# Attention, top-1 experts and a tanh layer in one kernel: all head pairs of a middle tile merged, softmax sums divided out later, weight splits moved

## The reference

```
# 1. attention: q, k, v of (4 batches, 8 heads, 768 rows, 64)
scores = q @ k.T / 8
keep   = (column < 4) | (0 <= row - column < 128)     # 4 sink keys, window of 128
a      = softmax(where(keep, scores, -1e9))           # + 1e-9 in the denominator
x      = (a @ v), heads side by side                  # 3072 x 512
# 2. one of 8 experts for each row
logits = x @ w_gate ; e = argmax(logits)
x      = softmax(logits)[e] * (relu(x @ w1[e]) @ w2[e])   # 512 -> 1024 -> 512
# 3. for all rows
h      = x @ w_in ; out = (h - tanh(h)) @ w_out       # 512 -> 2048 -> 512
```

## Time and profile before

| what | value |
|---|---|
| median of 3 runs | 1098.68 us (1098.45 to 1098.95) |
| the profiled execution's own time | 1091.45 us |
| its span in the profile | 1089.7 us |
| TensorE clock granted | 0.999 of full speed |
| busy in the span | PE 99%, PE weight loads 80%, DVE 56%, ACT 44%, POOL 44% |

### The profile page before, as it was taken

The page is one execution under the profiler, slowest core; times in us unless marked ns, Lnnn a source line. Parts: engine busy times, 40 slices in busy tenths (PEclk is TensorE's granted clock), DMA queues, the critical chain, the costliest instruction groups (busy, mean ns, idle before and its releaser), DMA issues.

```text
span 1089.7 us, 17185 instructions
## 1 busy us (share of the span) xinstructions
PE 1077.8 (99%) x6028; PEld 876.7 (80%) x6028; DVE 610.5 (56%) x1354; ACT 481.6 (44%) x1033; POOL 484.0 (44%) x492
## 2 busy tenths in 40 slices
PE   9999999999999999999999999999999999999997
PEld 6777876888888888888878888888888888888885
DVE  7778775233222332223378766666666666666664
ACT  7899875333142424442454433333333333333332
POOL 3265634715043617482264444345335335334532
PEclk9999999999999999999999999999999999999999
DMA  8646824516134434463231100101001011000000
GB/s 292 204 120 230 260 81 153 196 49 203 39 94 158 130 132 156 132 225 125 92 110 53 57 22 19 30 11 40 20 20 39 2 38 39 1 1 11 30 1 38
DMA packets 38204, 99.44 MB, mean 91 GB/s; under 512 B 8304, under 2 KB 8944, under 8 KB 33008
## 3 DMA queue, kind: packets, MB, share of 16 engines
q1 hardware_dynamic: 29392, 52.04, 15.4%
q0 software_dynamic: 8448, 46.17, 12.3%
q10 hardware_dynamic: 288, 0.26, 0.1%
HBM read 75.84 MB, written 22.61 MB: 90 GB/s over the span
## 4 chain that ended last, share of the span: by engine, by line
PE 97%; DVE 1%; issue 1%; ACT 1%; POOL 0%; POOLq 0%; ACTq 0%; DVEq 0%
PE bank L775 24%; PE bank L783 23%; PE bank L714 15%; PE bank L700 14%; PE bank L480 5%; PE bank L512 4%; PE bank L494 3%; PE bank L706 2%; PE bank L459 1%; PE bank L675 1%; PE bank L759 1%; PE bank L558 1%; PE bank L544 1%; PE bank L536 1%; DVE probT L1089 0%
## 5 line engine op out<-in xcount | busy, mean ns | idle before, releaser
L1521 POOL TENSOR_TENSOR weights<-raw,weights 128x1024 fp32r<-128x1024 f32 x70 | 166.6, 2400 | 199.3 <-ACT weights L843 198.2
L783 PE MATMUL bank<-weights,gT_hi 128*128 128x512 f32 x768 | 238.6, 392 | 0.3 <-DVE gT_lo L1388 0.3
L775 PE MATMUL bank<-mT_hi,weights 128*128 128x512 f32 x768 | 189.8, 389 | 0.7 <-ACT mT_hi L997 0.7
L1620 POOL TENSOR_SCALAR ser<-ser 128x512 f32<-128x512 f32 x96 | 61.8, 643 | 281.5 <-DVE ser L1333 281.4
L775 PEld LDWEIGHTS bank<-mT_hi,weights 128*128 128x128 f32 x768 | 144.1, 188 | 30.8 <-ACT mT_hi L997 0.9
L783 PEld LDWEIGHTS bank<-weights,gT_hi 128*128 128x128 f32 x768 | 142.6, 188 | 29.4 <-DVE gT_lo L1388 0.7
L783 PE MATMUL bank<-weights,gT_lo 128*128 128x512 f32 x384 | 149.6, 390 | 0.0
L1011 ACT ACTIVATE bank<-bank 128x512 f32<-128x512 f32 x96 | 55.9, 582 | 210.4 <-DVE ser L1364 210.4
L714 PE MATMUL bank<-weights,hT_hi 128*128 128x512 f32 x464 | 148.6, 401 | 0.0
L700 PE MATMUL bank<-weights,mT_hi 128*128 128x512 f32 x456 | 144.2, 397 | 0.0
L1622 POOL TENSOR_SCALAR sq<-sq 128x512 f32<-128x512 f32 x94 | 140.6, 1496 | 0.0
(11 more groups left out here) (164 smaller groups left out, 1593.7 us busy)
## 6 DMA issues: line engine op xcount, KB each, us to landing
raw<-w_all POOLq DMA_DIRECT2D x32, 1024.0 KB, 5.5
raw<-w_all SPq DMA_DIRECT2D x8, 1024.0 KB, 6.4
sorted_y<-ys SPq DMA_DIRECT2D x30, 257.0 KB, 4.2
xs<-sorted_x SPq DMA_DIRECT2D x29, 257.0 KB, 3.0
v_in<-vt SPq DMA_DIRECT2D x24, 256.0 KB, 3.9
kT<-kt SPq DMA_DIRECT2D x23, 264.0 KB, 3.1
qT<-qt SPq DMA_DIRECT2D x23, 256.0 KB, 4.1
raw<-sorted_y SPq DMA_DIRECT2D x20, 257.0 KB, 2.7
```

The source lines that it names most:

```text
L775: done = e.matmul(bank[HB[n % 3]][:, :], wt[:, f // 2, c, cols], x[:, c, :], start=(m == 0), stop=(m == 3 * CH - 1))
L783: done = e.matmul(bank[YB[i]][:, :], x[:, n % 3, rows], wt[:, f, :], start=(f == 0 and m == 0), stop=(f == GCH - 1 and m == 2))
L1521: e.tensor_tensor(lo, src, hi.bitcast(F32), ALU.subtract).then_inc(s_w_lo, 1)
L1620: e.tensor_scalar(row, row, SERIES_2, 1.0, ALU.mult, ALU.add).then_inc(s_ser, 1)
```

## The change

1. `is_merged` now holds for all four pairs of the middle tiles but those of tiles 22 and 23, which keep the old form; `part_on_act` is left for the second tile of a batch and for tiles 22 and 23. Semaphore counts follow from these functions.
2. `x_tok` gets the unscaled rows, by one ACT copy for each tile (`x_copy`), and the eight reciprocals beside them (columns `META` to `ROW`). A row in memory is 522 numbers long instead of 514. In the expert slots DVE multiplies `xs` by its reciprocals in place (`scale_x`), at the start of the slot before, and PE waits for that instead of for the load. `ys` carries ones in these columns, so that the rows loaded from `sorted_y` are multiplied by one.
3. The splits of expert 0 move: `hi` two at a time in steps 6, 12 and 18, `lo` in steps 7, 8, 13, 14, 19, 20, and the last two of each after the attention. Raw weights of expert 1 are loaded in steps 16, 17 and 23, the last quarter by POOL after the attention.
4. The product into `bank[MARK]` and the waits on `s_expert` are gone.

```
     def part_on_act(g, p):
         t = g % TILES
-        return t > 0 and p % 2 == 1
+        return t > 0 and p % 2 == 1 and not is_merged(g, p)
     def is_merged(g, p):
-        return g % TILES > 1 and p % 2 == 0
+        return g % TILES > 1 and (p % 2 == 0 or g < ALL - 2)
...
+    HI_IN, LO_IN, RAW_AT = (6, 6, 12, 12, 18, 18), (7, 8, 13, 14, 19, 20), (16, 17, 23)
...
+            def x_copy(w):                                     # ACT
+                if w >= RING_X:
+                    b = set_of[w - RING_X]
+                    e.wait_ge(scattered[b], 16 * SETS[b][1])
                 e.wait_ge(s_x_turned, w + 1)
...
+                e.activation(x_tok[:, w % RING_X, 0:DM], bank[T_OF[turn_at["x", w, 0] % 2]][:, :],
+                             ACT.Copy).then_inc(s_x_copied, 1)
...
                 if w >= 0:
                     logits_evict(w)
+                    x_copy(w)
                 if g >= 0:
                     o_evict(g)
                 if part_on_act(i, 1):
                     part(i, 1)
-                if 7 <= i < 15:
-                    split_hi(0, i - 7)
+                for y, at in enumerate(HI_IN):
+                    if at == i:
+                        split_hi(0, y)
...
-            normalise(ALL - 2)
+            x_copy(ALL - 2)
             route_exp(MULTI + 2)
-            normalise(ALL - 1)
+            x_copy(ALL - 1)
+            for y in range(len(HI_IN), 8):
+                split_hi(0, y)
...
                 if w >= 0:                                     # DVE, attention
-                    normalise(w)
                     add_logits(w)
...
+            def scale_x(heads):                                # DVE, experts
+                x = xs[:, heads.start * D:heads.stop * D].rearrange("p (h d) -> p h d", d=D)
+                each = xs[:, META + heads.start:META + heads.stop]
+                return e.tensor_tensor(x, x, each.unsqueeze(2).broadcast_to([P, heads.stop - heads.start, D]), ALU.mult)
             def slot_body():
+                e.wait_ge(x_loaded, r["next16"])
+                scale_x(slice(0, H)).then_inc(x_scaled, 1)
                 e.wait_ge(h_first, r["this"])
...
+            e.wait_ge(x_loaded, 16)
+            scale_x(slice(0, H // 2)).then_inc(x_half, 1)
+            scale_x(slice(H // 2, H)).then_inc(x_scaled, 1)
...
+            for y in range(len(LO_IN), 8):                     # POOL, after the attention
+                split_lo(0, y)
+            for j in range(len(RAW_AT), 4):
+                e.wait_ge(s_w_lo, 2 * j + 2)
+                load_raw(1, j)
...
-                e.wait_ge(x_loaded, r["next16"])               # PE, slot
+                e.wait_ge(x_scaled, r["next"])
                 turn_slot_x()
...
-                e.matmul(bank[MARK][0:1, 0:1], ident[:, 0:1], ident[:, 0:1], start=True, stop=True).then_inc(s_expert, 1)
...
-                else:
-                    e.wait_ge(s_expert, nxt - 1)
```

More of the change, by code:

```diff
@@ L34, in build @@
     REG = N + P
-    ROW = DM + 2
+    META = DM + 2
+    ROW = META + H
     SC = float(D) ** -0.5
@@ L50, in build @@
     IN_POOL = 5
+    HI_IN, LO_IN, RAW_AT = (6, 6, 12, 12, 18, 18), (7, 8, 13, 14, 19, 20), (16, 17, 23)
     QW = 2048
-    ZEROS_AT = 676
+    ZEROS_AT = 596
     HW = QW // 2
@@ L232, in build @@
         s_tail_rows = sem("tail_rows")
-        s_w_hi, s_w_lo, s_out_lo, s_expert = sem("w_hi"), sem("w_lo"), sem("w_out_lo"), sem("expert_done")
+        s_w_hi, s_w_lo, s_out_lo = sem("w_hi"), sem("w_lo"), sem("w_out_lo")
         s_in_lo = sem("w_in_lo_by_vector")
         s_m_hi_dve = sem("m_hi_by_vector")
+        x_half, x_scaled = sem("slot_x_half"), sem("slot_x_scaled")
         x_turned, x_hi, x_split = sem("slot_x_turned"), sem("slot_x_hi"), sem("slot_x_split")
@@ L445, in bank_of_turn @@
                     was, wg_, wp = turns[n - 2]
[L446 to L449, removed]
+                    if was == "x":
+                        e.wait_ge(s_x_copied, wg_ + 1)
                     elif part_on_act(wg_, wp):
@@ L666, in tensor, with turn_slot_x @@
             keep_warm(42, bank[R_BANK])
-            r = {n: e.alloc_register(f"pe_{n}") for n in ("this", "next16", "trips")}
+            r = {n: e.alloc_register(f"pe_{n}") for n in ("this", "next", "trips")}
             e.reg_mov(r["this"], 1)
-            e.reg_mov(r["next16"], 32)
-            def turn_slot_x():
+            e.reg_mov(r["next"], 2)
+            def turn_slot_x(first=False):
                 for c in range(CH):
+                    if first and c == CH // 2:
+                        e.wait_ge(x_scaled, 1)
                     done = e.transpose(bank[MT][:, c * P:(c + 1) * P], xs[:, c * P:(c + 1) * P], ident[:, :])
@@ L738, in slot_body @@
                 e.reg_add(r["this"], r["this"], 1)
-                e.reg_add(r["next16"], r["next16"], 16)
-            e.wait_ge(x_loaded, 16)
+                e.reg_add(r["next"], r["next"], 1)
+            e.wait_ge(x_half, 1)
             e.wait_ge(s_sums, 2)
-            turn_slot_x()
+            turn_slot_x(first=True)
             for _ in range(5):
@@ L838, in split_hi @@
                 src, hi, _ = w_half(n, x)
-                if n < 2:
+                late = x // 2 >= len(RAW_AT)
+                if n == 0 or (n == 1 and not late):
                     e.wait_ge(raw_in[x // 2], 16 * (n + 1))
                 else:
-                    e.wait_ge(raw_sw[x // 2], 16 * (n - 1))
+                    e.wait_ge(raw_sw[x // 2], 16 * (n if late else n - 1))
                 e.activation(hi, src, ACT.Copy).then_inc(s_w_hi, 1)
@@ L1106, in normalise @@
                     e.wait_ge(scattered[b], 16 * SETS[b][1])
[L1107 to L1111, removed]
+                e.wait_ge(s_rsum, g + 1)
+                e.reciprocal(x_tok[:, g % RING_X, META:ROW], rsum[:, g % 2, :]).then_inc(s_rinv, 1)
             def add_logits(w):
@@ L1273, in vector @@
             e.tensor_copy(offs[:, :], sums[:, 1, 3:3 + E]).then_inc(s_offs, 1)
-            r = {n: e.alloc_register(f"dve_{n}") for n in ("this", "next", "this16", "trips")}
+            r = {n: e.alloc_register(f"dve_{n}") for n in ("this", "next", "this16", "next16", "trips")}
             e.reg_mov(r["this"], 1)
```

47 lines of the change are left out of this document (15 added, 32 removed).

## The result

The changed kernel took 1100.74 us (median of 12 executions, 1099.19 to 1102.42), the kernel before 1098.53 beside it: a ratio of 1.0022, 95% interval 1.0013 to 1.0031. It is 2.2 us slower, where 3.0 us less was forecast. The profiled execution took 1100.52 us, its span is 1098.8 and the granted clock 0.995 of full speed.

What follows compares the result with a forecast made beforehand. PE's own queue was taken to bound the kernel. The terms, 5.9 - 1.2 - 2.4 + 0.5 - 0.8 - 0.6 + 1.6, gave 3.0 us less, from 1098.68 to 1095.7 us, range 1090.7 to 1099.5.

Steps and rivals of the forecast that it cites:

- blocks, loop through DVE and ACT: Attention: fewer turned blocks save PE 5.9 us; the loop through DVE and ACT, 6.9 us a step, loses 1.2.
- distances that end in steps 8, 14, 20: Attention steps where DVE was late: its missing division gives 0.5 us back in all, bounds 0 to 1.
- POOL's merges between scatters: Steps 10, 11, 16, 17: two more POOL merges beside scatters stall PE; 0.8 us lost, bounds 0 and 1.6.
- two ACT splits in steps 7, 13, 19: Two ACT splits at a time delay exponentials, and PE waits for the logits' copy; 2.4 us lost, bounds 1.5 to 3.0.
- `lo` splits beside the sinks' V split: Attention: POOL's 2.4 us splits at step ends without scatters, ahead of a merge that waits anyway; cost nothing.
- first slot: First expert slot: late load and scaling held by POOL's split delay relu and PE; 0.6 us lost, bounds 0 and 2.9.
- marks and last slot: Expert slots: dropping the mark products saves 0.2 us for each of eight; 1.6 us, between 1.0 and 2.9.
- The signs: Named evidence: 6.9 us middle steps, three `lT` waits of 0.7 to 1.0, filler over the seam, no gap between slots.
- the other slots that do not grow: Expert slots after the first: a scaling held by one 2.4 us split still ends in time; nothing, 28 times.
- PE gets all it saves: Rival, attention: ACT's and DVE's delays vanish in unseen gaps; 8.0 us less, 1090.7; chance 0.17.
- the loop keeps the old period: Rival, attention: costlier hand-overs keep middle steps at 7.2 us; 1098.9, no change; chance 0.24.
- The slower rival: Rival, expert slots: scaling held over two POOL splits makes relus late; 8 us lost, 1103.7; chance 0.13.

Runs made afterwards that it cites:

- experiment 11: The changed kernel, with POOL issuing its late raw load and starting expert weight splits only after DVE scaled x for slot 2; 1091.47 us, ratio 0.9999.
- experiment 2: The changed kernel with POOL's `lo` splits in steps 8, 9, 14, 15, 20, 21, away from DVE's sinks' V splits; 1095.98 us, ratio 0.9978.
- experiment 5: As experiment 2, with pair 0's product with V moved ahead of the second score group; 1096.18 us, ratio 0.9958.
- experiment 3: The changed kernel with all weight splits and raw loads back in the steps of the kernel before; 1099.48 us, ratio 1.0009.
- experiment 8: As experiment 5, plus the slot's scaling behind the first relu and the weight splits spread over single steps; 1098.17 us, ratio 0.9992.
- experiment 9: The changed kernel with splits spread and, in most steps, pair 0's values ahead of the second score group; 1085.63 us, ratio 0.9943.
- experiment 10: As experiment 9, with POOL starting expert splits only when `xs` of slot 2 is scaled; 1085.29 us, ratio 0.9941.
- experiment 12: The kernel before with one POOL `lo` split moved from step 12 onto step 13; 1092.79 us, ratio 1.0012.
- experiment 7: As experiment 2, with only the even pairs merged, as in the kernel before; 1097.61 us, ratio 0.9981.
- experiment 4: The kernel before without the mark product and the waits on `s_expert`; 1095.84 us, ratio 0.997.

## Why the prediction was wrong

The sum, term by term. Attention terms are from experiment 11 against the first profile of the kernel before, step by step; the others from the profiles named.

| term | forecast, us | measured, us |
|---|---|---|
| blocks, loop through DVE and ACT | -5.9 + 1.2 = -4.7 | -1.6, with POOL's |
| distances that end in steps 8, 14, 20 | -0.5 | -1.6, with those that end in 9, 15, 21 |
| POOL's merges between scatters | +0.8 | in the first row; 0.1 can be seen (step 11: 7.09, others 6.99) |
| two ACT splits in steps 7, 13, 19 | +2.4 | +0.71 + 0.67 + 0.77 = +2.15 |
| `lo` splits beside the sinks' V split | 0 | +4.5 |
| first slot | +0.6 | +4.15 (0.2 in experiment 11) |
| marks and last slot | -1.6 | -2.3 in the slots, -0.5 behind the last |
| end, after PE's last product | 0 | -1.0 |

The measured column comes to 3.8 more, the two profiles differ by 3.5 and the medians by 2.2. The first slot doesn't cost the same in each execution, which may be why: in two profiles with the same code from the attention's end on it was 14.28 (experiment 2, the load of `xs` there after 3.6 us) and 18.2 (experiment 5, after 4.5 us), and the five times of experiment 5 lie in two groups, 1091.9 to 1092.4 and 1096.2 to 1097.6. The end behind PE's last product is 6.4 us in the six profiles in which POOL makes the last raw load of expert 1 after the attention, and 7.4 in the eight in which it does not, experiments 3, 8, 9 and 10 among them; how the two hang together was not found.

**The step that failed** is the sentence on the `lo` splits, which stand "at the ends of steps in which no scatter is due, ahead of a merge that has to wait": nothing. For POOL's own queue that was right. But it asked only who waits for POOL, not what DVE has in the same place. Step 13 was the one step that the kernel before left out of `LO_AT` between 8 and 16, and in it DVE splits the sinks' V with two SBUF operands. The part on the first slot used the row that shows this hold and its 0.54 us; the attention's part did not. Experiment 2 takes the cost away (4.5 us in the steps), experiment 12 puts it into one step of the kernel before (8.71 us for 7.44).

The Trainium skill ("SBUF — State Buffer", section "Who interferes with whom") has the rule: a DVE instruction with two SBUF inputs contends with a GpSimd one that reads SBUF, and whoever comes second is fully blocked. The trace agrees, with 2.17 us for 0.68; the prediction had weighed this rule in the slots, and not in the attention.

**The second is a size: the first slot.** The mechanism (late landing, held scaling, relu behind it) was forecast, with bounds of 0 and 2.9 us. 0.6 was taken because most loads take 2.9 us. This one load is not like most: it is issued 3 us after a raw load of 1 MB that the change itself puts there, and it took 5.0. The upper bound lacked the clock: over a stall of 2.54 us PE's clock fell to 0.50, which made it into 4.0. Experiment 5 has the same with 2.52; stalls of 1.68 and 1.60 at this place in the second slots of experiments 9 and 7 left the clock at full speed.

**The third is the merging itself.** A middle step took 6.99, within 0.1 of the forecast of 6.9 (whose terms add up to 6.85, by which the loop would bind by 0.07 and not 0.12). But the loop was seen at the wrong place: what holds the step is mostly the second score group, which DVE frees late, as experiment 5 shows (6.87 with the order changed). So 0.21 of 0.42 us was got in a middle step. Of the fourteen tiles that lose blocks, six give almost nothing: the distances from t = 2 steps to the next are as long without the merging (8.05 in experiments 2 and 7, but for the first batch's), and so are those from t = 5 steps (6.22 and 6.23 at step 6). The merging gave some 1.6 us, POOL's stalls taken off, where 4.7 - 0.8 = 3.9 were forecast; with the splits of experiment 2 it gave 0.9. The total hides this, because the distances that end in steps 8 and 9, 14 and 15, 20 and 21 gained 1.6 us where 0.5 were forecast. Experiment 7 has this gain without the merging; DVE's missing division is its likely source, which no run tests alone.

**The signs** named in the prediction could not warn of this. Middle steps of 6.99, the three waits for `lT`, the filler over the seam and the slots without growth all came as forecast, and none of them looks at steps 8, 14 and 20.

**Right**: the ACT splits (2.4 against 2.15, at the three places named; with the splits on single steps the distance is back at 6.26), the filler that covers the seam, and the other slots that do not grow. POOL's stall, taken as 0.8, was some 0.1, inside its bounds.

**The rivals.** "PE gets all it saves" and "the loop keeps the old period" both fell as told, with middle steps of 6.99 between 7.20 and 6.78; but in the sum the merging gave 1.6 us, which is near the 1.5 of the second. The slower rival came true as a hold (over two splits: 4.95 us at 202.32 in experiment 11), but not as its price: ahead of the first relu it has twelve products as cover, and only a landing of 5 us together with two splits breaks through (1.9 us in one slot of experiment 9). What made the change slower was the same hold at a place that no rival named.

## What to carry to other kernels

When work is moved to another step, look in that step at the engines that share something with the moved one, not only at those that wait for it: here a DVE instruction with two SBUF operands ended 0.54 us after the POOL pass beside it, whatever its own length. An edit may be bound to its schedule (experiment 3), so a loss is looked for in where its parts were put, before the edit is given up: the changed kernel with other steps and pair 0's values moved forward is 0.6% faster than the kernel before (experiments 9 and 10). What an edit gives is best read from a run without it: the missing marks are 0.3% of this (experiment 4), and the merging, in experiment 7, was worth 0.9 us. And the median of a transfer's time is no estimate for the one transfer that starts beside another.

## What the runs showed of the hardware

- A DVE instruction that is held beside one POOL split ends 0.54 us after it (100.89 and 100.35). Beside two splits back to back it is held over both or only over the first. Over both: it ends 0.56 to 0.57 us after the second (experiment 11: 207.27 and 206.70; experiment 9: 203.10 and 202.54). Over the first alone, DVE and POOL in the changed kernel:

```profile
211.58 2.29 DVE L1280 TENSOR_TENSOR xs<-xs 128x512 f32<-128x512 f32 x1 [0.72 <-DMA xs<-sorted_x]
```

```profile
210.91 5.21 POOL L1526 TENSOR_TENSOR weights<-raw,weights 128x1024 fp32r<-128x1024 f32 x2 [1.42 <-ACT weights L842]
```

  DVE ends at 213.87, 0.56 after the first split (213.31), and the second split takes 2.84 us instead of 2.4. In the fourteen traces the hold covers both splits 72 times and the first alone 19 times. The 19 are those in which ACT's `hi` split, for which POOL's second split waits, ended only after POOL's first had begun; in the 72 it had ended before. Why this decides it was not tested. The prediction had "until POOL was done", from a single instruction.
- The order of the records does not settle who is held. In experiment 9 the scaling begins at 197.38, 0.41 us before POOL's split, while POOL still issues its load (197.19, 0.57 us), and is held all the same; in experiment 7 too (209.57 and 210.03).
- An instruction with one small operand can be caught as well: the `TENSOR_SCALAR` of 128x8 at 188.20 took 5.37 us and ended at 193.57, beside a scatter and two splits of POOL that ended at 193.54. In the same place of the kernel before it took 0.17. It is hidden by filler.
- The same program took 1098.5 us on one chip and 1091.8 on another, 0.6% less. The traces show a pause of PE, DVE and ACT of 2.6 us, a slow clock after it and a few smaller waits. It need not be the chip alone: the first profiled execution of the kernel before lacks the pause too (1091.45 us), beside runs of 1098.7. What is behind the pause was not found.
